# A short bias table, sums shared between two engines, first MLP products in the last attention pair, and identity products on TensorE

## The chip, the cores and the metric

The kernel runs on one core of a Trainium2 chip. The metric is the device time of one execution in microseconds (us), smaller is better. TensorE (PE in the rows) multiplies; PEld is its weight load. VectorE (DVE), ScalarE (ACT) and GpSimd (POOL) work element by element, SyncE (SP) issues transfers. Each has its own instruction stream, executed in order; they meet at semaphores.

## What is computed

A banded attention followed by two MLPs, all in float32. The reference, cut:

```python
# q, k, v: (2, 8, 768, 64); n_global 8, n_local 96
scores = scale * q @ k^T - slope[head] * dist       # dist: distance in the band, n_local for the global columns
scores = where(is_global | is_local, scores, -1e9)
x = softmax(scores) @ v                              # then (1536, 512)
h = x @ w_in                                         # w_in (512, 2048)
x = (h * tanh(softplus(h))) @ w_out                  # w_out (2048, 512)
for e in range(4):                                   # 4 experts, w1 (512, 1024), w2 (1024, 512)
    out += p[:, e:e+1] * (relu(x @ w1[e]) @ w2[e])
```

## The kernel before

**Attention** takes about the first sixth of the time. Its 16 heads form 8 pairs; a pair has 12 units, one for each of 6 blocks of 128 queries and each head, so there are 96 units, counted 0 to 95. Unit `u` goes through five steps:

1. scores: PE, `scores_of_two` (L535), for two units at once, three units ahead of the unit in hand. For the first block of queries a unit has 128 key columns, for the second 256, for the others 288.
2. bias, scale and running minimum: DVE, `biased` (L1074), two units ahead. It adds the table `dist_b` that `band_tables` (L1047) makes at the start: distance to the key plus a huge negative number where the key is masked.
3. exponential: ACT, `expo` (L824), two units ahead.
4. transpose: PE, `turn` (L566), then a high part by ACT (L858) and a low part by DVE (L1184).
5. product with the values: PE, `pv` (L585), two units behind.

After 6 units the outputs are divided by their sums and stored in `acc` (DVE, `output`, L1106 to L1114). While a pair runs, q and k of the next are transposed: PE, `fill` (L497), in four parts at units 0, 2, 4 and 6 of the pair, each copied out of one PSUM bank by ACT (`copy_out`, L814 and L817). The order is q tiles 0 to 3, q tiles 4 and 5, k tiles 0 to 3, k tiles 4 and 5. Before unit 0 the same is done for pair 0, and its scores wait for all four copies.

Beside this, in the same streams: DVE takes the largest absolute value of the values of each pair (`value_step`, L1155, units 0 to 6) and makes a scale from it (unit 7). ACT sums the absolute values of `w_in` in 8 pieces of 128x1024 at units 21 to 28, and of `w_out` at units 33 to 40 (`weights_sum`, L841). DVE makes scales of these (`matrix_scale`), and POOL splits both matrices into two float16 parts (L745 to L751).

**The first MLP** has 48 steps T (3 groups g of 512 tokens, 16 blocks of w_in columns). `first_product(T)` is 12 products of 128x512 (L635) in bank T % 4. Then ACT and DVE form the activation: ACT L939; DVE L1297, L1299, L1303 on the same T; ACT L953, L955 and DVE L1315, L1317 on T-1; POOL L790; ACT L947 and DVE L1309 on T-2. `second_product(T - 4)` is 12 products (L658). Before all this PE transposes the attention output: for g = 0 inside the last four pairs, for g = 1 and 2 in `turn_x` (L505, 16 transposes), at the steps that the table `TURN_AT` gives; ACT and DVE then take high and low parts (ACT L893, DVE `x_low`, L1169, 4 each). `second_product(0)` writes to the banks that `turn_x` used, so it waits until all of `x_low` is done. `first_product(0)` waits for the last `output` of attention. The experts follow.

The order in every stream is written out in the program; nothing is rearranged.

Of the kernel before, what the change touches and what calls it, by code (L numbers as in the profile page):

```python
# [13 lines left out]
P = 128  # L14
# [22 lines left out]
def program(nc, q, k, v, n_global, n_local, w_in, w_out, probs, w1, w2, out):  # L37
# [35 lines left out]
    with ExitStack() as ctx:  # L73
# [103 lines left out]
        dist_b, key_b, loc_b = (scratch(BAND_COLS) for _ in range(3))  # L177
# [5 lines left out]
        rel_b, glo_b = dist_b, tmp[:, 3 * BAND_COLS:4 * BAND_COLS]  # L183
# [56 lines left out]
        w_piece = sem("w_piece")  # L240
# [56 lines left out]
        TURN_AT = {0: 1, 2: 2}  # L297
# [39 lines left out]
        FILL = [(j, t) for j in range(2) for t in (range(HEAD), range(HEAD, QT))]  # L337
# [38 lines left out]
        def run_attention(eng, first, pair, rest):  # L376
# [18 lines left out]
            with eng.If(banded == 1):  # L395
                run(True)
                rest()
            with eng.Else():
                run(False)
                rest()  # L400
# [79 lines left out]
        def _(pe):  # L480
            def fill(i, slot, k, banded):
# [14 lines left out]
                for n, t in enumerate(tiles):  # L496
                    last = pe.transpose(psum(k if m_0 else 3, P, n * P), nat[slot][j][:, t * P:(t + 1) * P], ident[:])  # L497
# [10 lines left out]
            def score_parts(i, slot, u, banded):  # L508
# [3 lines left out]
                if u == 0:  # L512

                    pe.wait_ge(tr_out, FILLS * (2 * i + slot + 1))
# [73 lines left out]

            def pair(i, slot, banded):
                for u in range(UNITS):  # L590
# [34 lines left out]
            def rest():  # L625

                pe.wait_ge(o_ready, 2 * PAIRS + 2)

                def split_product(dst, lhs, rhs, chunks, fresh=None):

                    for c in range(chunks):
                        if fresh is not None:
                            fresh(c)
                        for n, (a, b) in enumerate(((0, 0), (0, 1), (1, 0))):
                            last = pe.matmul(dst, lhs(c, a), rhs(c, b), start=(c == 0 and n == 0),  # L635
                                             stop=(c == chunks - 1 and n == 2))
                    return last

                def first_product(T):

                    g, f = divmod(T, FT)
                    if T >= 4:
                        pe.wait_ge(b_ready, T - 3)
                    split_product(psum(T % 4), lambda c, s: w_in_s[:, s, c, f * P:(f + 1) * P],
                                  lambda c, s: xs(g, c, s), DC).then_inc(h_psum, 1)
# [51 lines left out]
                pe.wait_ge(x_ready, DC)  # L697
                pe.wait_ge(w_split, 1)
                for T in range(STEPS + LAG):
                    if T < STEPS:  # L700
# [3 lines left out]
                    if T in TURN_AT:  # L704
                        pe.wait_ge(x_ready, DC * TURN_AT[T])
# [13 lines left out]
            pe.wait_ge(ident_ready, 1)  # L719
            for k in range(FILLS):  # L720
# [85 lines left out]
        def _(act):  # L806
# [27 lines left out]
            def weights_sum(n, c):  # L834
# [3 lines left out]
                if n + c:  # L838
                    act.wait_ge(w_piece, PIECES * n + c)
                src = w_out_raw if n else stage  # L840
                act.activation(scaled[:], src[:, c * PIECE:(c + 1) * PIECE], ACT.Abs,  # L841
                               accum_out=wpieces[:, c:c + 1]).then_inc(w_piece, 1)
# [7 lines left out]
            def pair(i, slot, banded):  # L850
                for u in range(UNITS):
# [568 lines left out]
```

## Time and profile before

| what | us |
|---|---|
| median of 3 runs (lowest, highest) | 916.49 (912.8, 917.21) |
| the profiled execution, its own time | 915.88 |
| its span in the trace | 913.8 |
| attention, until the last product with the values | 153 |
| from there to `first_product(5)` | 24 |
| the rest, MLP and experts | 737 |

The trace was taken from one execution. In a row, a time in us comes first, then the duration, the engine, the line, the operation and the tiles; what stands in brackets is the idle time of the engine just before it and what ended that. The granted clock of PE (PEclk) is 1.00 at 2.4 GHz and 0.50 at 1.2 GHz. Float32 products are seen twice in the trace for each one in the program.

### The profile page before, as it was taken

The numbers are of one execution on the slowest core, as the hardware profiler recorded it, in microseconds if no ns is written. First come the engines' busy times: TensorE is split into PE (matmuls) and PEld (weight loads), VectorE is DVE, ScalarE is ACT, GpSimd is POOL, SyncE is SP. The second block draws the span as 40 slices with busy tenths as digits, with TensorE's granted clock in tenths as the row PEclk, the third lists the DMA queues.
The fourth block names the chain that finished last, engine by engine and source line by source line (L and its number), as shares of the span: only waits on it lengthen the run. The fifth ranks groups of instructions, "written<-read, shape, count | busy, mean of one in ns | idle before, by whom it ended". The sixth has DMA issues, their size and how long they took to land.

```text
span 913.8 us, 12568 instructions
## 1 busy us (share of the span) xinstructions
PE 873.1 (96%) x4884; PEld 441.3 (48%) x4884; DVE 506.8 (55%) x1016; ACT 315.7 (35%) x591; POOL 266.0 (29%) x218
## 2 busy tenths in 40 slices
PE   3878998999999999999999999999999999999998
PEld 3766786444444444444444444444444444444443
DVE  7855876999999999996642225322134322212121
ACT  3699885545454555454030111101020101101020
POOL 1266994122222232320009500059000193000000
PEclk8798999999999999999999999999999999999999
DMA  9762340000000000202000400000400000000001
GB/s 220 242 220 55 82 156 1 1 1 1 0 1 10 1 0 1 78 18 93 4 6 0 151 34 0 7 1 2 182 1 0 6 0 0 1 24 23 34 12 49
DMA packets 52005, 39.20 MB, mean 43 GB/s; under 512 B 40816, under 2 KB 41712, under 8 KB 51440
## 3 DMA queue, kind: packets, MB, share of 16 engines
q1 hardware_dynamic: 49888, 34.31, 12.5%
q10 hardware_dynamic: 2064, 4.19, 1.3%
q8 instruction: 31, 0.51, 0.3%
q14 instruction: 22, 0.18, 0.1%
HBM read 35.35 MB, written 3.15 MB: 42 GB/s over the span
## 4 chain that ended last, share of the span: by engine, by line
PE 69%; DVE 21%; ACT 7%; issue 2%; DMA 0%; POOL 0%; DVEq 0%; SPq 0%; ACTq 0%
PE bank L635 58%; PE bank L658 5%; DVE tmp L1299 4%; DVE tmp L1317 3%; PE bank L540 2%; DVE xT L1315 2%; DVE tmp L1297 2%; PE bank L566 2%; DVE tmp L1303 2%; ACT scaled L841 2%; PE bank L585 1%; DVE hid L1309 1%; ACT tmp L824 1%; ACT tmp L858 1%; ACT tmp L953 1%
## 5 line engine op out<-in xcount | busy, mean ns | idle before, releaser
L927 ACT ACTIVATE hid<-bank 128x512 f16<-128x512 f32 x96 | 57.3, 596 | 410.6 <-PE bank L635 410.6
L635 PE MATMUL bank<-xT,wA 128*128 128x512 f16 (+1 forms) x864 | 196.2, 381 | 1.1 <-DVE acc L1114 1.1
L1290 DVE SCALAR_TENSOR_TENSOR hid<-bank,hid 128x512 f16<-128x512 f32 x96 | 66.4, 692 | 172.3 <-ACT hid L927 172.3
L658 PE MATMUL bank<-hid,wB 128*128 128x512 f16 x576 | 132.2, 379 | 4.4 <-ACT acc L911 2.6
L635 PEld LDWEIGHTS bank<-xT,wA 128*128 128x128 f16 x864 | 84.8, 98 | 103.7 <-issue 2.2
L790 POOL TENSOR_TENSOR tmp<-tmp 128x512 f32<-128x512 f32 x48 | 70.1, 1460 | 198.2 <-DVE tmp L1317 198.2
L635 PE MATMUL bank<-wA,hid 128*128 128x512 f16 x576 | 125.3, 379 | 0.0
L635 PE MATMUL bank<-xT,wB 128*128 x576 | 125.3, 379 | 0.0
L635 PE MATMUL bank<-wB,hid 128*128 128x512 f16 x576 | 125.3, 379 | 0.0
L745 POOL TENSOR_SCALAR stage<-stage,sc 128x1024 f32<-128x1024 f32 x32 | 35.9, 1120 | 252.8 <-DVEq L1283 240.8
L1366 DVE SCALAR_TENSOR_TENSOR acc<-bank,pg,acc 128x512 f32<-128x512 f32 x36 | 27.0, 751 | 131.7 <-PE bank L635 131.7
L658 PEld LDWEIGHTS bank<-hid,wB 128*128 128x128 f16 x576 | 56.1, 98 | 73.0 <-DVE hid L1309 3.6
L635 PEld LDWEIGHTS bank<-wA,hid 128*128 128x128 f16 x576 | 56.4, 98 | 67.9
L635 PEld LDWEIGHTS bank<-xT,wB 128*128 128x128 f16 x576 | 56.4, 98 | 68.0
L635 PEld LDWEIGHTS bank<-wB,hid 128*128 128x128 f16 x576 | 56.4, 98 | 68.0
L947 ACT ACTIVATE hid<-tmp 128x512 f16<-128x512 f32 x48 | 30.2, 630 | 107.8 <-POOL tmp L790 106.0
L1184 DVE SCALAR_TENSOR_TENSOR tmp<-bank,tmp 128x384 f16<-128x384 f32 (+2 forms) x96 | 47.0, 490 | 30.5 <-ACT tmp L858 29.4
L635 PE MATMUL bank<-xT,hid 128*128 (+1 forms) x288 | 63.3, 379 | 0.0
L824 ACT ACTIVATE tmp<-tmp 128x288 f32<-128x288 f32 (+2 forms) x96 | 48.7, 507 | 20.3 <-DVE tmp L1074 18.8
L566 PE MATMUL bank<-ident,tmp 128*128 128x128 f32 x240 | 47.4, 299 | 6.0 <-DVE tmp L1184 3.3
L1299 DVE SCALAR_TENSOR_TENSOR tmp<-tmp 128x512 f32<-128x512 f32 x48 | 48.4, 1007 | 1.6
L540 PE MATMUL bank<-hid 64*128 64x256 f32 (+2 forms) x320 | 39.7, 360 | 9.1 <-DVE tmp L1074 8.2
(110 smaller groups left out, 930.6 us busy)
## 6 DMA issues: line engine op xcount, KB each, us to landing
stage<-in_moe_w SPq DMA_DIRECT2D x8, 2048.0 KB, 9.1
stage<-in_moe_w_in SPq DMA_DIRECT2D x1, 4096.0 KB, 14.2
wB<-in_moe_w_out ACTq DMA_DIRECT2D x1, 4096.0 KB, 15.9
hid<-in_q SPq DMA_DIRECT2D x16, 192.0 KB, 3.2
hid<-in_k SPq DMA_DIRECT2D x16, 192.0 KB, 3.4
xT<-in_v SPq DMA_DIRECT2D x8, 384.0 KB, 5.1
out_y<-acc SPq DMA_DIRECT2D x12, 256.0 KB, 2.0
rows<-max SPq DMA_DIRECT2D x4, 128.0 KB, 4.2
```

What stands on the lines that cost most here:

```text
L540: last = pe.matmul(*parts[a][n], start=True, stop=True)
L566: last = pe.transpose(dst[:, b * P:(b + 1) * P], src[:, b * P:(b + 1) * P], ident[:])
L635: last = pe.matmul(dst, lhs(c, a), rhs(c, b), start=(c == 0 and n == 0), stop=(c == chunks - 1 and n == 2))
L658: last = pe.matmul(psum(4 + d), w_out_s[:, a, f // 2, f % 2, d * P:(d + 1) * P], hv[:, T % RING, b, :], start=(f == 0 and n == 0), stop=(f ...
L745: pool.tensor_scalar(tmp, src, scale, 1.0, ALU.mult, ALU.mult).then_inc(w_part, 1)
L790: pool.tensor_tensor(g_t[T % 4], g_t[T % 4], r_t[T % 2], ALU.mult).then_inc(g_ready, 1)
L824: act.activation(t, t, ACT.Exp, bias=nmax[:, u:u + 1], scale=-1.0).then_inc(p_ready, 1)
L927: act.activation(hv[:, f, 0, :], psum(f % 4), ACT.Relu).then_inc(f_hi, 1)
L947: act.activation(hv[:, m % RING, 0, :], g_t[m % 4], ACT.Copy).then_inc(h_hi, 1)
L1184: dve.scalar_tensor_tensor(pt[:, 1], src, P_SCALE, pt[:, 0], ALU.mult, ALU.subtract).then_inc(pT_dve, 1)
L1290: dve.scalar_tensor_tensor(hv[:, f, 1, :], psum(f % 4), 0.0, hv[:, f, 0, :], ALU.max, ALU.subtract).then_inc(f_ready, 1)
L1299: dve.scalar_tensor_tensor(n, u, 2.0, u, ALU.add, ALU.mult).then_inc(n_ready, 1)
```

## The change

- **Short table.** `band_tables` loses its helper `distances`: one operation of 128x672 and three memsets of the score buffers now stand ahead of the wait for `bounds`, and four operations of 128x672 behind it where there were eight.
- **Start.** PE multiplies the identity 13 times (`keep_busy`) as soon as it exists. `FILL` now orders its parts q 0 to 3, k 0 to 3, q 4 and 5, k 4 and 5 (in every pair), and the scores of pair 0 wait only for the first two copies. `biased` of unit 2 is moved ahead of the value scale; `value_step(0)` ahead of the low part of the values.
- **Shared sums.** Of the 8 pieces of each weight matrix ACT keeps the even ones, DVE takes the odd ones (`weights_part`, one reduction of 128x1024). Of the 7 reductions of values DVE keeps four, and ACT takes those of pairs 3, 5 and 7 at units 2, 4 and 6.
- **First MLP products in the last pair.** At units 9, 10 and 11 of pair 7 PE does half of `first_product(0)`, its other half, and half of `first_product(1)`, 6 products each. The wait for the last `output` is moved from ahead of the MLP to ahead of `turn_x`. `TURN_AT` puts the transposes of g = 1 behind step 1 (was 0) and those of g = 2 behind step 3 (was 2).
- **Identity products.** In `scores_of_two` for units 6 to 46 PE multiplies the identity by itself three times, behind the waits of the scores and ahead of the scores, in the bank that the scores then overwrite: 21 places, 63 products.

```diff
-        dist_b, key_b, loc_b = (scratch(BAND_COLS) for _ in range(3))
+        dist_b, key_b = (scratch(BAND_COLS) for _ in range(2))
...
-        TURN_AT = {0: 1, 2: 2}
+        TURN_AT = {1: 1, 3: 2}
+        EARLY = [(0, (0, 1)), (0, (2, 3)), (1, (0, 1))]
...
+        V_SUMS = list(range(3, PAIRS, 2))
         W_SUMS = ({0: 21, 1: 33}, {0: UNITS})
+        BUSY = range(6, W_SUMS[0][1] + PIECES + 6)
...
-        FILL = [(j, t) for j in range(2) for t in (range(HEAD), range(HEAD, QT))]
+        FILL = [(j, t) for t in (range(HEAD), range(HEAD, QT)) for j in range(2)]
...
-                if u == 0:
-
+                if banded and before(i, slot) is None:
+                    if u in (0, 2 * HEAD):
+                        pe.wait_ge(tr_out, 2 if u == 0 else FILLS)
+                elif u == 0:
                     pe.wait_ge(tr_out, FILLS * (2 * i + slot + 1))
...
                 parts = [score_parts(i, slot, u + a, True) for a in range(2)]
+                if (2 * i + slot) * UNITS + u in BUSY:
+                    for _ in range(3):
+                        pe.matmul(psum(u % 3, P), ident[:], ident[:], start=True, stop=True)
...
+            def keep_busy(times):
+                for _ in range(times):
+                    pe.matmul(psum(3, P), ident[:], ident[:], start=True, stop=True)
...
                     scores_of_two(0, 0, 2)
+                    keep_busy(3)
...
+                        if not after(i, slot) and u >= UNITS - len(EARLY):
+                            n = u - (UNITS - len(EARLY))
+                            if n == 0:
+                                pe.wait_ge(x_ready, DC)
+                                pe.wait_ge(w_split, 1)
+                            first_product(*EARLY[n])
                         if behind:
                             pv(*behind, banded)
...
-                pe.wait_ge(o_ready, 2 * PAIRS + 2)
...
                 for T in range(STEPS + LAG):
-                    if T < STEPS:
+                    if banded and T < 2:
+                        if T:
+                            first_product(1, (2, 3))
+                    elif T < STEPS:
                         first_product(T)
                     else:
                         expert_first(0, 0, T - STEPS)
                     if T in TURN_AT:
+                        pe.wait_ge(o_ready, 2 * PAIRS + 2)
                         pe.wait_ge(x_ready, DC * TURN_AT[T])
...
             pe.wait_ge(ident_ready, 1)
+            keep_busy(13)
...
-                        if start <= at < start + PIECES:
+                        if at - start in range(0, PIECES, 2):
...
+                    if at + 1 in V_SUMS:
+                        values_sum(at + 1)
...
+            dve.wait_ge(iotas, 3)
+            dve.scalar_tensor_tensor(rel_b, rel_b, -1.0e9, rel_b, ALU.mult, ALU.max)
+            for s in s_b:
+                last = dve.memset(s[:, 2 * P + GLOBAL_COLS:3 * P], 0.0)
+            link(last)
...
-                distances(link, rel_b, key_b, loc_b, glo_b)
-                link(dve.tensor_scalar(loc_b, loc_b, -1.0, 1.0e9 * 2 ** H / SCALE, ALU.add, ALU.mult))
-                dve.scalar_tensor_tensor(dist_b, rel_b, -1.0 / SCALE, loc_b, ALU.mult, ALU.add).then_inc(band_ready, 1)
+                link(dve.tensor_scalar(key_b, key_b, bf[:, 0:1], -1.0e9 * 2 ** H / SCALE, ALU.is_ge, ALU.mult))
+                link(dve.scalar_tensor_tensor(key_b, rel_b, bf[:, 1:2], key_b, ALU.is_ge, ALU.mult))
+                link(dve.tensor_scalar(rel_b, rel_b, bf[:, 1:2], -1.0 / SCALE, ALU.min, ALU.mult))
+                dve.tensor_tensor(dist_b, rel_b, key_b, ALU.add).then_inc(band_ready, 1)
...
+                    if first is not None and at - first in range(1, PIECES, 2):
+                        weights_part(n, at - first)
```

On PE, the end of attention and the beginning of the MLP. `bank<-ident,tmp` is `turn`, the 128x65 products are `pv`, `bank<-xT,wA` is `first_product`, `bank<-ident,acc` is `turn_x`, `bank<-hid,wB` is `second_product`. Before:

```order
L566 MATMUL bank<-ident,tmp 128x128 x3
L585 MATMUL bank<-xT,tmp 128x65 x27
L635 MATMUL bank<-xT,wA 128x512 x12
L505 MATMUL bank<-ident,acc 128x128 x16
L635 MATMUL bank<-xT,wA 128x512 x24
L505 MATMUL bank<-ident,acc 128x128 x16
L635 MATMUL bank<-xT,wA 128x512 x24
L658 MATMUL bank<-hid,wB 128x512 x12
```

Now, from unit 9 of the last pair on:

```order
L581 MATMUL bank<-ident,tmp 128x128 x3
L610 MATMUL bank<-xT,wA 128x512 x6
L600 MATMUL bank<-xT,tmp 128x65 x9
L581 MATMUL bank<-ident,tmp 128x128 x3
L610 MATMUL bank<-xT,wA 128x512 x6
L600 MATMUL bank<-xT,tmp 128x65 x27
L610 MATMUL bank<-xT,wA 128x512 x6
L509 MATMUL bank<-ident,acc 128x128 x16
L610 MATMUL bank<-xT,wA 128x512 x24
L509 MATMUL bank<-ident,acc 128x128 x16
L610 MATMUL bank<-xT,wA 128x512 x12
L679 MATMUL bank<-hid,wB 128x512 x12
```

Three half products moved in among the last units, and of the products that stood behind the second `turn_x` only one is left behind it.

On ACT, from unit 20 to 24, where the pieces of `w_in` are summed. Before:

```order
L858 ACTIVATE tmp<-bank 128x384
L824 ACTIVATE tmp<-tmp 128x288
L841 ACTIVATE scaled,wpieces<-stage 128x1024
L858 ACTIVATE tmp<-bank 128x384
L824 ACTIVATE tmp<-tmp 128x128
L841 ACTIVATE scaled,wpieces<-stage 128x1024
L858 ACTIVATE tmp<-bank 128x384
L824 ACTIVATE tmp<-tmp 128x128
L841 ACTIVATE scaled,wpieces<-stage 128x1024
```

Now:

```order
L893 ACTIVATE tmp<-bank 128x384
L852 ACTIVATE tmp<-tmp 128x288
L868 ACTIVATE scaled,wpieces<-stage 128x1024
L893 ACTIVATE tmp<-bank 128x384
L852 ACTIVATE tmp<-tmp 128x128
L893 ACTIVATE tmp<-bank 128x384
L852 ACTIVATE tmp<-tmp 128x128
L868 ACTIVATE scaled,wpieces<-stage 128x1024
```

Every second piece left this stream; it stands in DVE's, behind the low part (L1237 now) of the same unit.

On PE, at unit 13, the scores of units 16 and 17 (`bank<-hid`). Before:

```order
L497 MATMUL bank<-ident,hid 128x128 x4
L566 MATMUL bank<-ident,tmp 128x128
L540 MATMUL bank<-hid 128x256 x2
L540 MATMUL bank<-hid 128x32 x2
L585 MATMUL bank<-xT,tmp 128x65 x9
```

Now:

```order
L501 MATMUL bank<-ident,hid 128x128 x4
L581 MATMUL bank<-ident,tmp 128x128
L546 MATMUL bank<-ident 128x128 x3
L549 MATMUL bank<-hid 128x256 x2
L549 MATMUL bank<-hid 128x32 x2
L600 MATMUL bank<-xT,tmp 128x65 x9
```

The three identity products stand between the transpose of the unit and the scores; everything behind them in the stream comes later by their length, if PE had no wait there.

## Rows read from the trace of the kernel before

**Rows 1.** The page, part 1: busy time, share of the span, instructions.

```profile
PE 873.1 (96%) x4884; PEld 441.3 (48%) x4884; DVE 506.8 (55%) x1016; ACT 315.7 (35%) x591; POOL 266.0 (29%) x218
```

**Rows 2.** Timeline, start of the program: start, duration, engine, line, operation, idle before.

```profile
3.03 0.28 DVE L1005 TENSOR_SCALAR ident<-tmp 128x128 f32<-128x128 f32 x1
...
6.61 0.51 DVE L1040 TENSOR_SCALAR tmp<-tmp 128x672 f32<-128x672 f32 x1 [1.04 <-issue]
7.15 0.92 DVE L1041 SCALAR_TENSOR_TENSOR tmp<-tmp,bf 128x672 f32<-128x672 f32 x1
...
7.63 2.79 PE L497 MATMUL bank<-ident,hid 128*128 128x128 f32 x12 [7.63 <-DMA hid<-in_k]
...
10.95 0.49 PE L540 MATMUL bank<-hid 64*128 64x128 f32 x4 [0.52 <-ACT hid L817]
...
12.34 0.86 DVE L1052 SCALAR_TENSOR_TENSOR tmp<-tmp 128x672 f32<-128x672 f32 x1
...
13.87 0.29 DVE L1074 CUSTOM_DVE_ANT_0 tmp<-bank,tmp 128x128 f32<-128x128 f32 x1 [0.23 <-DVE tmp L1384]
```

**Rows 3.** Groups of 0 to 154 us by form: count, busy us, mean ns, idle before.

```profile
L841 ACT ACTIVATE scaled<-stage 128x1024 f32<-128x1024 f32 x8 | 8.5, 1056 | 0.0
...
L1155 DVE TENSOR_REDUCE vpart<-xT 128x1 f32<-128x768 f32 x7 | 6.6, 943 | 0.0
```

**Rows 4.** Timeline, DVE, low part of units 12, 21, 29, 33 and 41.

```profile
40.43 0.29 DVE L1184 SCALAR_TENSOR_TENSOR tmp<-bank,tmp 128x128 f16<-128x128 f32 x1 [0.64 <-ACT tmp L858]
...
51.59 0.55 DVE L1184 SCALAR_TENSOR_TENSOR tmp<-bank,tmp 128x384 f16<-128x384 f32 x1
...
66.54 0.56 DVE L1184 SCALAR_TENSOR_TENSOR tmp<-bank,tmp 128x384 f16<-128x384 f32 x1 [0.91 <-ACT tmp L858]
...
71.22 0.55 DVE L1184 SCALAR_TENSOR_TENSOR tmp<-bank,tmp 128x384 f16<-128x384 f32 x1
...
87.06 0.56 DVE L1184 SCALAR_TENSOR_TENSOR tmp<-bank,tmp 128x384 f16<-128x384 f32 x1 [0.91 <-ACT tmp L858]
```

**Rows 5.** Timeline, PE: one float32 product, and the same scores two pairs apart.

```profile
69.86 0.47 PE L547 MATMUL bank<-ident,sc 128*128 128x128 f32 x2
70.16 0.49 PE L566 MATMUL bank<-ident,tmp 128*128 128x128 f32 x3
...
110.63 0.84 PE L540 MATMUL bank<-hid 64*128 64x256 f32 x8
...
139.37 0.84 PE L540 MATMUL bank<-hid 64*128 64x256 f32 x8
```

**Rows 6.** Stretches: from:to, length, PE busy (records), granted clock, DMA share, GB/s.

```profile
24.00:26.00 2.00, 2.00 (x21) 0.50 0.44 98
...
80.00:82.00 2.00, 2.00 (x8) 0.50 0.04 8
...
96.20:139.30 43.10, 40.65 (x525) 1.00 0.36 117
```

**Rows 7.** Timeline, PE and DVE, end of attention to step 5 of the MLP.

```profile
152.53 0.43 PE L585 MATMUL bank<-xT,tmp 128*128 128x65 f16 x9 [0.49 <-DVE tmp L1184]
...
154.04 4.43 PE L635 MATMUL bank<-xT,wA 128*128 128x512 f16 x12 [1.08 <-DVE acc L1114]
...
159.29 0.43 DVE L1297 TENSOR_SCALAR tmp<-tmp 128x512 f32<-128x512 f32 x1 [5.05 <-ACT tmp L939]
...
171.54 2.48 DVE L1169 TENSOR_TENSOR xT<-bank,xT 128x512 f16<-128x512 f32 x4
...
174.08 2.76 PE L658 MATMUL bank<-hid,wB 128*128 128x512 f16 x12 [1.75 <-DVE xT L1169]
...
176.68 2.75 PE L635 MATMUL bank<-xT,wA 128*128 128x512 f16 x12
...
177.65 0.42 DVE L1297 TENSOR_SCALAR tmp<-tmp 128x512 f32<-128x512 f32 x1
...
182.50 0.42 DVE L1297 TENSOR_SCALAR tmp<-tmp 128x512 f32<-128x512 f32 x1
```

More of the change, by code:

```diff
@@ L496, in fill @@
                 for n, t in enumerate(tiles):
-                    last = pe.transpose(psum(k if m_0 else 3, P, n * P), nat[slot][j][:, t * P:(t + 1) * P], ident[:])
+                    last = pe.transpose(psum(4 + k if m_0 else 3, P, n * P), nat[slot][j][:, t * P:(t + 1) * P], ident[:])
                 last.then_inc(tr_psum, 1)
@@ L587, in pv, with split_product, first_product @@
                 last.then_inc(pv_done, 1)
+            def split_product(dst, lhs, rhs, chunks, fresh=None, only=None):
+                for c in only or range(chunks):
+                    if fresh is not None:
+                        fresh(c)
+                    for n, (a, b) in enumerate(((0, 0), (0, 1), (1, 0))):
+                        last = pe.matmul(dst, lhs(c, a), rhs(c, b), start=(c == 0 and n == 0),
+                                         stop=(c == chunks - 1 and n == 2))
+                return last
+            def first_product(T, only=None):
+                g, f = divmod(T, FT)
+                if T >= 4:
+                    pe.wait_ge(b_ready, T - 3)
+                last = split_product(psum(T % 4), lambda c, s: w_in_s[:, s, c, f * P:(f + 1) * P],
+                                     lambda c, s: xs(g, c, s), DC, only=only)
+                if not only or DC - 1 in only:
+                    last.then_inc(h_psum, 1)
             def pair(i, slot, banded):
@@ L623, in pair, with rest @@
                     share_max(1)
-            def rest():
-                pe.wait_ge(o_ready, 2 * PAIRS + 2)
[L629 to L645, printed above, removed]
+            def rest(banded):
                 def second_product(T):
@@ L883, in pair @@
                     act.wait_ge(w_max, 1)
-                    for c in range(PIECES):
+                    for c in range(0, PIECES, 2):
                         weights_sum(1, c)
@@ L893, in x_high, with rest @@
                 act.activation(xs(g, c, 0), psum(x_bank(g, c)), ACT.Copy).then_inc(x_hi, 1)
-            def rest():
+            def rest(banded):
                 def x2_high(g, c):
@@ L1150, in value_step @@
             def value_step(u):
-                if u + 1 < PAIRS:
-                    n = u + 1
+                n = u + 1
+                if n < PAIRS and n not in V_SUMS:
                     dve.wait_ge(v_loaded[n], 16)
@@ L1178, in pair @@
                         biased(i, slot, u, banded)
-                    elif ahead:
+                    elif ahead and ahead != (0, 0, 2):
                         biased(*ahead, banded)
@@ L1208, in attention @@
                                   apply_absolute_value=True).then_inc(v_max, 1)
+                if is_banded:
+                    biased(0, 0, 2, is_banded)
                 dve.wait_ge(v_amax, 1)
@@ L1211, in attention @@
                 dve.sem_inc(v_scale, 1)
+                value_step(0)
                 values_low(0)
-                pair(0, 0, is_banded, value_step)
+                pair(0, 0, is_banded, lambda u: u and value_step(u))
                 pair(0, 1, is_banded, lambda u: matrix_step(1, u, is_banded))
@@ L1378, in _ @@
             with dve.If(banded == 1):
-                link = chain(table_step)
-                dve.wait_ge(iotas, 3)
-                band_tables(link)
+                band_tables(chain(table_step))
                 dve.wait_ge(band_ready, 1)
-                for s in s_b:
-                    last = dve.memset(s[:, 2 * P + GLOBAL_COLS:3 * P], 0.0)
-                link(last)
                 attention(True)
@@ L1392, in _ @@
                 dve.sem_inc(tables_free, 1)
+                for c in range(1, PIECES, 2):
+                    weights_part(1, c)
                 weights_max(1)
```

45 lines of the change are left out of this document (29 added, 16 removed).

## The prediction, made before the changed kernel ran

> **What bounds the kernel now.** I read the page's busy times first. TensorE is busy for 873 of 914 us [rows 1]; the change touches nothing behind step 5 of the MLP, at 177 us, and from there PE runs without a break. So the question is only how much earlier or later `first_product(5)`, now at 176.68 [rows 7], begins. I then read the timeline of the first 180 us and, beside it, the stretches with PE's granted clock. The reader is to see four different limits.
>
> In the start (0 to 14 us) DVE is the limit: PE could score at 10.95, DVE takes up the first scores at 13.87, when its table is done [rows 2]. In pair 0 DVE and a PE at 1.2 GHz share it: in 24 to 26 us PE is busy all the time at 0.50 [rows 6]. In the units in which weights are summed ACT is the limit: DVE waits 0.91 us for ACT's copy at units 29 and 41 [rows 4]. From pair 4 on PE is: two pairs take 28.74 us, 14.37 each or 2.40 for two units [rows 5], and PE is busy for 40.65 of 43.10 us [rows 6]. At the beginning of the MLP DVE is the limit: `second_product(0)` waits 1.75 us for `x_low` [rows 7].
>
> **Start and pair 0.** Removed behind the wait for the bounds: four of eight table operations. What is left is 0.51 + 0.92 + 0.51 + 0.86 = 2.80 us [rows 2], about 2.95 with gaps, instead of 7.26 (6.61 to 13.87). The operation put ahead costs 0.86, and the memsets are there too; half of it fits in DVE's wait for the bounds, the rest delays the flag by an estimated 0.3. DVE could take scores at 6.9 + 2.95 + 0.3 = 10.2. Now PE is late: 13 products seen twice are 26 records; the first 12 transposes took 2.79 us, 0.23 each [rows 2], so from 3.35 they last until 8.5 to 9.4, while k landed at 7.6. Eight transposes and two copies by ACT follow; scores at 10.2 to 11.3, DVE at 10.7 to 11.7. I take 10.9: -3.0 us.
>
> Then DVE loses three reductions, 3 x 0.94 = -2.8 [rows 3], which ACT gets, and PE gets five calls of the identity products. What one call costs: the one full float32 product of the trace holds PE for 0.30 us from its start to the next (69.86 to 70.16), of which some is the step over to it; as a stream two records of 128 columns should take 0.22, as transposes do. So 0.66 a call, 0.90 at most at full clock, about double at half clock, and nothing where PE waits anyway. Five calls: +3.3, partly under waits for DVE. If they keep the clock up they return more than that: PE is at 0.50 in much of pair 0 [rows 6]. The net from this to unit 14 I put at -2.0 (+1 to -4). Together **-5.0** (-2 to -7).
>
> Here the row and a rule meet. PE was busy for 2.00 of 2.00 us at a granted 0.50 in 24 to 26 us, with transposes among its records [rows 6]. The Trainium skill (TensorE: Matmul & The Clock Gate, Part 4: PE-mode transpose) says that a transpose does not count as busy for the clock as a plain product does. By that rule the identity products do what the transposes don't, the clock is up from an early call on, and the term would be the -7 of its lower end, the forecast 2 us lower.
>
> **Shared sums, units 21 to 28 and 33 to 40.** Now 66.54 - 51.59 = 14.95 and 87.06 - 71.22 = 15.84 us, 30.8 for 16 units, 3.85 for two [rows 4]. Of two pieces (1.06 us each [rows 3]) ACT loses one: 2.79 for two units, if only ACT counted. PE needs 2.40 [rows 5] + 0.66 = 3.06. DVE gets one reduction of 128x1024, 0.94 x 1024/768 = 1.25, on top of what it does for two units; it is the chain's other link and not far below 3. Three engines with about the same load never run at the bare sum: I take 3.25, so 8 x 3.25 = 26.0: **-4.8** (22.3 with hidden products, -8.5; nothing gained, 0). What stretched 80 to 82 us (clock 0.50 [rows 6]) is in the 15.84.
>
> **Identity products elsewhere.** Of 21 calls 5 are in pair 0 and 8 in the units just counted. The other 8 (issued in units 13 to 19, 29, 31, 41 and 43) come where PE has no wait to hide them: 51.59 - 40.43 = 11.16 us for units 12 to 20 is 2.48 for two units, PE's own pace [rows 4, 5]. 8 x 0.66 = **+5.3** (0 to 7.2). Queued behind them on PE: scores, `pv` and the next `turn`; DVE and ACT wait for these.
>
> **First products in the last pair.** PE gets 18 products of 0.217 us (174.08 to 176.68 for 12 [rows 7]), 3.9 us, at units 9 to 11. I estimate its idle time there at 1.4 us, from pauses like the 0.49 before the last `pv` [rows 7], so the last `pv` ends 2.5 us later. Behind it the stream is shorter: `first_product(0)` at 154.04 took 4.43 us, at full clock it is 2.75 [rows 7]. But PE does not set the end of this stretch, DVE does. DVE began step 0 at 159.29, which is 6.3 us after the last `pv` (152.96). Now steps 0 and 1 are ready by then, and DVE begins 2.1 us after it (the last `output`, two scale operations, ACT's exponential): 152.96 + 2.5 + 2.1 = 157.6, 1.7 earlier. From there to the end of `x_low` for g = 2 DVE was busy nearly without a gap, 159.29 to 174.02, 14.7 us [rows 7]. `TURN_AT` moves those transposes from step 2 to step 3, so one more step of DVE's work stands ahead of them: in 14.7 us less two `x_low` of 2.48 stand two and a half steps, 3.9 each; later steps follow each other in 4.85 (177.65 to 182.50), waits included. I take 3.9. Then 157.6 + 14.7 + 3.9 = 176.2 instead of 174.02, +2.2. PE, which now ends `first_product(4)` some 7 us before, waits all that time instead of 1.75, and after such a pause restarts at 1.2 GHz, as it did at 154.04 after 1.08: 4.43 - 2.75 = +1.7. Together **+4.0** (if the last pair hides everything and the extra step costs half, -2; if the restart costs double, +5.7). Nothing later gives it back, since PE runs without a pause from `second_product(0)` on.
>
> POOL's splits come earlier with the units and are not waited for. The new `FILL` order moves two transposes from unit 4 to unit 2 of a pair: 0.
>
> **Sum.** -5.0 - 4.8 + 5.3 + 4.0 = -0.5: 915.88 becomes 915.4. The median lay 0.6 above the profiled execution, so 916.0.
>
> **Rivals.**
> 1. *The products hide* (faster). The scores are issued three units ahead, so a delay of 0.66 need not reach anyone; the sums then go at 2.8 to 3.0 for two units, pair 0 at full clock. -7 - 7.5 + 2 + 4 = -8.5: 908. For it: in the summing units PE waits. Against it: in pairs 4 to 6 PE has only 2.45 of 43.10 us free [rows 6].
> 2. *PE becomes the bound of pairs 0 to 3* (slower). A call costs 0.90 and every one of the 21 is paid; the sums gain only 2. Pair 0 -2, sums -2, elsewhere +7.2, MLP +5.5: +8.7, 925. It decides once a call is over 0.8 us and two units with sums over 3.6.
> 3. *The identity products do not raise the clock* (the change does not do what it says). Pair 0 and the region of 80 us stay at 0.50, where a call costs 1.3. Pair 0 -2, sums -2.5, elsewhere +5.3, MLP +4: +4.8, 921.
> 4. *The long wait ahead of `second_product(0)` does not come*, since ACT and DVE overlap the extra step: MLP -1 instead of +4, the rest as forecast: 911.
>
> **How the numbers follow.** Forecast 916 (912 to 920): 0.47. Rival 1, 908: 0.17. Rival 4, 911: 0.11. Rival 3, 921: 0.10. Rival 2, 925: 0.15. The range 908 to 923 leaves out half of rival 1 and most of rival 2. A measurement can tell about 0.5%, 4.6 us, from no change: below 911.9 lie rivals 1 and 4, faster 0.28; same 0.47; above 921.1 rival 2 and most of rival 3, slower 0.25.
>
> **What would show it.** The first `biased` at 10.7 to 11.7 us. Unit 12's low part at about 35.5 (40.43 now). Units 21 to 28 in 13 us, units 12 to 20 in about 14. No 0.50 in the stretches between 30 and 150 us. A call of six records lasting 0.6 to 0.7 us. The wait of `second_product(0)` for `x_low` grown to about 7 us with the clock at 0.50 behind it, and `first_product(5)` at 176. I am wrong if the scores come no later for the calls, if the extra step of DVE is hidden, or if the clock falls in spite of them.

## The result, and the profile after

| | before | after |
|---|---|---|
| median, us (lowest, highest) | 915.96 (912.8, 917.21), 7 runs | 921.77 (921.2, 923.99), 7 runs |
| profiled execution, its own time | 915.88 | 922.25 |
| its span | 913.8 | 920.4 |

The changed kernel takes 1.0076 times as long, with a 95% interval of 1.0060 to 1.0091: slower by 7 us. The forecast was 916.0, no change. The time lies above the 912 to 920 that stood beside the forecast and inside the wider range of 908 to 923; the slowdown itself was missed.

In the profile after, lines 1237, 1123, 852, 893 and 868 are what 1184, 1074, 824, 858 and 841 were before. New are L1074 (a piece of a weight matrix, reduced by DVE) and L546 (the identity products). Part 1 of the page answers [rows 1]:

```profile
PE 885.5 (96%) x5042; PEld 456.4 (50%) x5042; DVE 504.7 (55%) x1018; ACT 312.7 (34%) x581; POOL 265.3 (29%) x218
```

PE has 158 records more, 126 of them the identity products ahead of the scores and 32 those at the start, and is busy for 12 us more. DVE and ACT have less to do than before, so no busy time says where the 7 us went. The timeline of the start answers [rows 2] (start, duration, engine, line, operation, idle before):

```profile
3.37 5.00 PE L562 MATMUL bank<-ident 128*128 128x128 f32 x26 [3.37 <-DVE ident L1042]
...
10.73 0.29 DVE L1123 CUSTOM_DVE_ANT_0 tmp<-bank,tmp 128x128 f32<-128x128 f32 x1 [0.85 <-PE bank L549]
```

The first scores are taken up at 10.73 instead of 13.87. The low parts of units 12, 21, 29, 33 and 41 answer [rows 4]:

```profile
36.51 0.29 DVE L1237 SCALAR_TENSOR_TENSOR tmp<-bank,tmp 128x128 f16<-128x128 f32 x1 [0.26 <-ACT tmp L893]
...
49.27 0.56 DVE L1237 SCALAR_TENSOR_TENSOR tmp<-bank,tmp 128x384 f16<-128x384 f32 x1
...
66.08 0.55 DVE L1237 SCALAR_TENSOR_TENSOR tmp<-bank,tmp 128x384 f16<-128x384 f32 x1
...
71.58 0.55 DVE L1237 SCALAR_TENSOR_TENSOR tmp<-bank,tmp 128x384 f16<-128x384 f32 x1
...
89.59 0.55 DVE L1237 SCALAR_TENSOR_TENSOR tmp<-bank,tmp 128x384 f16<-128x384 f32 x1
```

Differences of such rows (DVE's low part of the first and the last unit named) give the table that every experiment below is read with. In us:

```
units            before   after   difference
0 to 14           23.93   23.93    0.00   (unit 0 itself: 19.55, now 15.62)
14 to 21           8.11    9.72   +1.61
21 to 29 (sums)   14.95   16.81   +1.86
29 to 33           4.68    5.50   +0.82
33 to 41 (sums)   15.84   18.01   +2.17
41 to 48           8.98   10.14   +1.16
48 to 95          55.80   57.36   +1.56   (early products in the last pair)
```

So of the 3.93 us won at unit 0 and still there at unit 14, 0.46 are left at unit 29, and unit 48 comes at 99.73 instead of 96.04. The units in which DVE and ACT now share the sums should have become 4.8 us shorter and became 4.0 us longer. The end of attention and the MLP's first steps on PE answer [rows 7]:

```profile
157.66 0.99 PE L600 MATMUL bank<-xT,tmp 128*128 128x65 f16 x27
158.49 1.46 PE L610 MATMUL bank<-xT,wA 128*128 128x512 f16 x6
...
179.14 5.30 PE L679 MATMUL bank<-hid,wB 128*128 128x512 f16 x12 [6.34 <-DVE xT L1222]
184.23 3.00 PE L610 MATMUL bank<-xT,wA 128*128 128x512 f16 x12
```

`second_product(0)` waits 6.34 us for `x_low`, where it waited 1.75, and its 12 products take 5.30 us, where 2.76 is full clock. The stretches from 176 us on (from:to, length, PE busy with its records, granted clock, DMA share, GB/s) show the clock at its lower level, 1.2 GHz, behind that pause:

```profile
176.00:178.00 2.00, 0.00 (x0) 0.97 0.00 0
178.00:180.00 2.00, 0.86 (x3) 0.50 0.00 0
180.00:182.00 2.00, 2.00 (x6) 0.50 0.01 4
```

`first_product(5)` begins at 184.23 instead of 176.68: 7.55 us late, of which 3.69 stem from before unit 48 and 3.86 from here.

**The ring.** Why did less work for ACT make the sum units longer? The chain of waits of both kernels tells it. Before, from 53.66 us on (start, us, what):

```profile
53.66 0.29 ACT tmp L824
53.95 1.04 ACT scaled L841 x2
54.99 0.37 ACT tmp L858
55.36 0.29 ACT tmp L824
55.65 1.04 ACT scaled L841 x2
```

The chain never leaves ACT: exponential, a piece (1.04), copy, 1.7 us a unit. After, the same stretch:

```profile
55.60 1.21 DVE wpieces L1074
56.81 0.26 issue
57.19 0.51 ACT tmp L852
57.70 0.57 ACT hid L842
58.27 1.04 ACT scaled L868 x2
59.31 0.28 ACT tmp L893
59.65 0.30 issue
59.96 1.21 DVE wpieces L1074
```

The chain now goes round between the two engines, and it holds DVE's piece and ACT's piece, one behind the other: 4.36 us for two units (55.60 to 59.96), 1.21 + 1.04 of it the two reductions. The timeline shows the two waits that close the ring:

```profile
57.19 0.51 ACT L852 ACTIVATE tmp<-tmp 128x256 f32<-128x256 f32 x1 [1.26 <-DVE tmp L1123]
...
58.17 1.05 ACT L868 ACTIVATE scaled<-stage 128x1024 f32<-128x1024 f32 x1
...
59.62 0.42 DVE L1237 SCALAR_TENSOR_TENSOR tmp<-bank,tmp 128x256 f16<-128x256 f32 x1 [1.81 <-ACT tmp L893]
...
59.96 1.21 DVE L1074 TENSOR_REDUCE wpieces<-stage 128x1 f32<-128x1024 f32 x1
```

In units 22, 24 and so on, those of the odd pieces, DVE's reduction stands ahead of `biased` for a unit ahead, and ACT idles for 1.26 us. In the unit between, ACT's piece stands ahead of its copy, and DVE idles for 1.81 us. Each engine does its piece while the other waits for it. Below this is called theory R (the ring). Its rival is theory P, that PE with its identity products is the bound.

### The profile page after: what moved, and what is told of

It is laid out like the page before. It is cut to its first block, busy times and chain, and to the rows that moved or that the text cites. A ratio compares the mean times of both kernels' runs of the same rounds, so it can differ in the third digit from the quotient of the medians.

```text
span 920.4 us, 12884 instructions
## 1 busy us (share of the span) xinstructions
PE 885.5 (96%) x5042; PEld 456.4 (50%) x5042; DVE 504.7 (55%) x1018; ACT 312.7 (34%) x581; POOL 265.3 (29%) x218
## 3 DMA queue, kind: packets, MB, share of 16 engines
HBM read 35.35 MB, written 3.15 MB: 42 GB/s over the span
## 4 chain that ended last, share of the span: by engine, by line
PE 84%; DVE 9%; ACT 4%; issue 2%; SPq 1%; DMA 0%; POOL 0%; DVEq 0%; ACTq 0%
PE bank L610 65%; PE bank L679 12%; PE bank L549 2%; PE bank L581 2%; PE bank L600 2%; DVE tmp L1353 1%; DVE tmp L1355 1%; ACT scaled L868 1%; ACT tmp L852 1%; PE bank L501 1%; ACT tmp L893 1%; DVE xT L1222 1%; SPq L418 1%; DVE tmp L1373 1%; DVE tmp L1359 1%
## 5 line engine op out<-in xcount | busy, mean ns | idle before, releaser
L679 PE MATMUL bank<-hid,wB 128*128 128x512 f16 x576 | 134.7, 384 | 7.8 <-DVE xT L1222 6.3
L773 POOL TENSOR_SCALAR stage<-stage,sc 128x1024 f32<-128x1024 f32 x32 | 35.9, 1123 | 253.3 <-DVEq L1339 241.0
L1237 DVE SCALAR_TENSOR_TENSOR tmp<-bank,tmp 128x384 f16<-128x384 f32 (+2 forms) x96 | 47.0, 490 | 28.5 <-ACT tmp L893 27.4
L976 ACT ACTIVATE tmp<-bank,sc 128x512 f32<-128x512 f32 x48 | 32.8, 685 | 56.4 <-PE bank L610 53.3
L581 PE MATMUL bank<-ident,tmp 128*128 128x128 f32 x240 | 44.6, 285 | 7.3 <-DVE tmp L1237 4.9
L1353 DVE TENSOR_SCALAR tmp<-tmp 128x512 f32<-128x512 f32 x48 | 39.5, 823 | 13.3 <-ACT tmp L976 13.2
## 6 DMA issues: line engine op xcount, KB each, us to landing
stage<-in_moe_w_in SPq DMA_DIRECT2D x1, 4096.0 KB, 14.7
```

The costliest lines, as they stand in the source:

```text
L581: last = pe.transpose(dst[:, b * P:(b + 1) * P], src[:, b * P:(b + 1) * P], ident[:])
L679: last = pe.matmul(psum(4 + d), w_out_s[:, a, f // 2, f % 2, d * P:(d + 1) * P], hv[:, T % RING, b, :], start=(f == 0 and n == 0), stop=(f ...
L773: pool.tensor_scalar(tmp, src, scale, 1.0, ALU.mult, ALU.mult).then_inc(w_part, 1)
L976: act.activation(u_t[T % 2], psum(T % 4), ACT.Exp, scale=inv_h).then_inc(u_ready, 1)
L1237: dve.scalar_tensor_tensor(pt[:, 1], src, P_SCALE, pt[:, 0], ALU.mult, ALU.subtract).then_inc(pT_dve, 1)
L1353: dve.tensor_scalar(u, u, U_MAX, None, ALU.min).then_inc(n_step, 1)
```

## The experiments

Kernels that were measured together share one set of runs of the kernel before. The ratio to that set is given with each, and kernels of different sets are compared by their ratios. The kernels whose names begin with a_ are the changed kernel with one part edited. The places of units are read from one trace of each kernel.

### Without the identity products ahead of scores (a_noident)

```diff
-        BUSY = range(6, W_SUMS[0][1] + PIECES + 6)
+        BUSY = range(0)
```

> The changed kernel without the 21 calls of three identity products ahead of scores; the 13 and the 3 of the start stay. Theory R (ring): in units 21 to 28 and 33 to 40 ACT's piece and DVE's reduction stand in units that follow each other and lie one behind the other in one ring of waits, so both are paid in full; the identity products are hidden there. Then these 16 units stay at 34.8 us, only the other stretches lose about 3.6, and the time is about 918. Theory P (PE): the identity products make PE the bound there too; the 16 units fall to 28 us or less and the time to 909 to 911.

Measured: 918.29 us, 1.0049 of before (1.0026 to 1.0072), span 915.1. The sum units took 16.79 and 17.99 us, as with the products (16.81, 18.01). Units 14 to 21, 29 to 33 and 41 to 48 took 8.03, 4.83 and 9.48, together 3.02 less. So the products are hidden where the ring turns and are paid in the other units behind unit 14; PE is not what made the sum units long, as theory R has it. Units 0 to 14 took 21.17 instead of 23.93; more on that under d_pair0.

### The same products alone, on the kernel before (b_ident)

```diff
                 parts = [score_parts(i, slot, u + a, True) for a in range(2)]
+                if (2 * i + slot) * UNITS + u in range(6, 47):
+                    for _ in range(3):
+                        pe.matmul(psum(u % 3, P), ident[:], ident[:], start=True, stop=True)
```

> The kernel before with nothing but the 21 calls of three identity products. Theory R: hidden in the 16 units, where ACT alone sums (30.8 us stay, less 1 or 2 if the clock stays up at 80 us); paid elsewhere, some 3.6 us in units 12 to 47 and 1 to 3 in pair 0 where PE runs at half clock; time about 920. Theory P: 16 units at 34 us or more, time 924 or above.

Measured: 918.42 us, 1.0046 (1.0026 to 1.0065), span 915.4. Sum units 14.96 and 15.85, unchanged. Units 0 to 14 +0.52, 14 to 21 +1.84, 29 to 33 +0.66, 41 to 48 +0.65: unit 48 at 99.72, 3.68 later. The edit costs the kernel before about as much up to unit 48 as the whole change does. Of those 3.7 us about 2 did not reach the end of the span (+1.6): `first_product(0)` ran at the upper clock there, 2.76 us for its 12 products where [rows 7] have 4.43. That need not come from the products. Behind the same wait of 1.07 or 1.08 us these 12 products took 4.43 to 4.45 us in three traces (before, a_noearly, d_start) and 2.76 or 2.77 in two (b_ident, d_noearly), and a_noearly has the identity products too.

### All pieces of the weights on ACT again (a_actsums)

```diff
-                        if at - start in range(0, PIECES, 2):
+                        if at - start in range(PIECES):
...
-                    if first is not None and at - first in range(1, PIECES, 2):
-                        weights_part(n, at - first)
```

> The changed kernel with all 16 pieces of the weight sums on ACT, as in the kernel before, and none on DVE; values stay shared, identity products stay. Theory R: the 16 units go back to the 30.8 us of before, time about 918. Theory P: with PE as the bound it makes no difference or is worse (ACT has more to do), 34.8 us or more, time 921 or above.

Measured: 917.39 us, 1.0036 (1.0025 to 1.0047), span 916.1. Sum units 15.07 and 15.97, within 0.13 of what they were before, with the identity products still there. Undoing the sharing alone gives back 3.7 us (1.0076 less 1.0036): the sharing is what costs, not what stands around it.

### DVE's piece in the same unit as ACT's (a_sameunit)

```diff
-                    if first is not None and at - first in range(1, PIECES, 2):
-                        weights_part(n, at - first)
+                    if first is not None and at - first in range(0, PIECES, 2):
+                        weights_part(n, at - first + 1)
```

> The changed kernel with DVE's reduction moved from the unit behind ACT's piece into the same unit, so that the two lie side by side. Theory R: the ring pays one of the two instead of both, 1.0 to 1.2 us less for two units; the 16 units take 26 to 28 us instead of 34.8, time about 914. Theory P: no change, 921.

Measured: 913.16 us, 1.0000 (0.9984 to 1.0016), span 911.2. Sum units 12.50 and 13.70: 26.2 us where the changed kernel has 34.8 and the kernel before 30.8. No operation was added or taken away; four pieces of each matrix moved by one unit. The timeline of this kernel shows the pieces side by side:

```profile
53.03 1.04 ACT L868 ACTIVATE scaled<-stage 128x1024 f32<-128x1024 f32 x1
53.07 1.21 DVE L1074 TENSOR_REDUCE wpieces<-stage 128x1 f32<-128x1024 f32 x1
...
55.56 1.21 DVE L1074 TENSOR_REDUCE wpieces<-stage 128x1 f32<-128x1024 f32 x1
...
56.19 1.05 ACT L868 ACTIVATE scaled<-stage 128x1024 f32<-128x1024 f32 x1
```

With the pieces side by side two units take 26.2 / 8 = 3.27 us. That is close to the 3.25 of the forecast, but not for the forecast's reason, which was the load of PE with its identity products. Up to unit 29 the chain of waits goes on between ACT and DVE, with one piece for two units instead of two, and enters PE only at 60.95 us, 0.9 us before the low part of unit 29. An estimate from the rows fits: the ring took 16.81 / 4 = 4.20 us for two units up to there, less ACT's piece of 1.05 that is 3.15; measured are 12.50 / 4 = 3.12. And c_three below, which has no identity products here, takes the same 12.50.

Of these 8.6 us, 7.6 arrive at unit 48 (92.09 for 99.73), since units 29 to 33 and 41 to 48 took 0.9 more. The ratio fell from 1.0076 to 1.0000, 7.0 us. The fall of the clock at 80 us is gone too: 1.00 from 74 to 90 us, where the changed kernel has

```profile
74.00:78.00 4.00, 2.20 (x30) 1.00 0.00 0
78.00:82.00 4.00, 3.95 (x30) 0.61 0.02 4
82.00:86.00 4.00, 4.00 (x23) 0.53 0.00 0
```

There PE was busy for 2.20 of 4.00 us, then the clock fell, in spite of the identity products among its records.

### The end of attention and the MLP as before (a_noearly)

```diff
-        TURN_AT = {1: 1, 3: 2}
+        TURN_AT = {0: 1, 2: 2}
-        EARLY = [(0, (0, 1)), (0, (2, 3)), (1, (0, 1))]
+        EARLY = []
...
+                pe.wait_ge(o_ready, 2 * PAIRS + 2)
...
-                    if banded and T < 2:
-                        if T:
-                            first_product(1, (2, 3))
-                    elif T < STEPS:
+                    if T < STEPS:
```

> The changed kernel with the end of attention and the start of the MLP as in the kernel before: no first products in the last pair, transposes behind steps 0 and 2. If the prediction's term for this part holds (+4.0 by its working), the wait for x_low is 1.75 us again, the clock stays up behind it, and the time is 3 to 4 us below the changed kernel, 918. Rival: the early products were worth something after all and the loss is only in attention: 921 to 923.

Measured: 919.45 us, 1.0044 (1.0031 to 1.0057), span 917.9. `first_product(5)` begins at 180.73, 3.5 us before that of the changed kernel:

```profile
158.08 4.45 PE L610 MATMUL bank<-xT,wA 128*128 128x512 f16 x12 [1.07 <-DVE acc L1160]
...
178.13 2.76 PE L679 MATMUL bank<-hid,wB 128*128 128x512 f16 x12 [1.74 <-DVE xT L1219]
180.73 2.75 PE L610 MATMUL bank<-xT,wA 128*128 128x512 f16 x12
```

The old order has its own fall of the clock (4.45 us for 12 products) and still gets there first. The wait is the 1.7 expected; the time lies between the 918 expected and the 921 of the rival.

### The second transposes behind step 2 (a_turn12)

```diff
-        TURN_AT = {1: 1, 3: 2}
+        TURN_AT = {1: 1, 2: 2}
```

> The changed kernel with the second group of transposes behind step 2 instead of step 3, early products kept. If the extra step of DVE ahead of x_low is what makes the long wait, the wait of 6.3 us ahead of second_product(0) is gone; instead PE waits some 4 us ahead of the second transposes (for the first x_low). first_product(5) comes 4.5 to 6.5 us earlier than at 184.2, time 915.5 to 917.5. Rival: the wait only moves ahead of the transposes in full and the clock falls there: 920 to 922.

Measured: 917.82 us, 1.0026 (1.0015 to 1.0037), span 916.1.

```profile
168.78 3.41 PE L509 MATMUL bank<-ident,acc 128*128 128x128 f32 x16 [3.98 <-DVE xT L1222]
171.99 5.58 PE L610 MATMUL bank<-xT,wA 128*128 128x512 f16 x24
177.41 2.75 PE L679 MATMUL bank<-hid,wB 128*128 128x512 f16 x12
180.00 2.75 PE L610 MATMUL bank<-xT,wA 128*128 128x512 f16 x12
```

The pause has moved ahead of the transposes and is 3.98 instead of 6.34 us. The slow clock behind it costs 1.5 us on the transposes (3.41 against 1.91), and `second_product(0)` waits for nothing. `first_product(5)` comes 4.2 us earlier, where 4.5 was the least expected, and the time is 0.3 above the range expected. The step that the change had put ahead of `x_low` is what the wait ahead of `second_product(0)` was made of; about 4 us of waiting for DVE are left, ahead of the transposes.

### PE kept at work through the wait (a_fillwait)

22 identity products into a free bank, in the pause ahead of `second_product(0)`:

```diff
                     if T == 0:
+                        pe.wait_ge(b_ready, 2)
+                        for _ in range(22):
+                            pe.matmul(psum(1, P), ident[:], ident[:], start=True, stop=True)
                         pe.wait_ge(x_ready, XN)
```

> The changed kernel with 22 identity products in the pause ahead of second_product(0). They take 22 x 0.28 = 6.1 us, what the pause lasts. If the fall of the clock in the pause costs what 5.30 instead of 2.75 us for its 12 products say, second_product(0) starts where it did (179.1) and first_product(5) 2.5 to 2.9 us earlier, time 919. Rival: identity products don't hold the clock in a pause, or the loss comes back later: 921 to 922.

Measured: 919.47 us, 1.0051 (1.0032 to 1.0070), span 917.9.

In this kernel L674 is the filler and L682 `second_product`. Its timeline:

```profile
172.75 5.07 PE L674 MATMUL bank<-ident 128*128 128x128 f32 x44
179.25 2.76 PE L682 MATMUL bank<-hid,wB 128*128 128x512 f16 x12 [1.43 <-DVE xT L1225]
181.85 2.75 PE L610 MATMUL bank<-xT,wA 128*128 128x512 f16 x12
```

The product starts no earlier (179.25, 179.14 in the changed kernel) but runs at the upper clock: the next begins 2.4 us earlier. So of the 3.86 us of this part about 2.4 are the clock behind the pause. The rest, about 1.4, is that `second_product(0)` itself begins later. The price of the clock is not a constant: behind the same wait of 6.33 us the 12 products took 5.30 us in a_noident, 4.93 in a_actsums and 4.33 in a_sameunit.

### Three edits together (c_three)

The edits of a_sameunit, a_noident and a_turn12 in one kernel.

> Three edits of the changed kernel together: reduction in the same unit as ACT's piece, no identity products ahead of scores, second transposes behind step 2. If the three are independent: 913.2 for the first, 4 to 5 less for the second, 4 to 6 less for the third, 903 to 905, below both kernels. Rival: without identity products ACT and DVE are the bound in the 16 units, or the clock falls in attention, and it is 907 to 910.

Measured: 904.83 us (903.92 to 907.0), 0.9892 of before (0.9862 to 0.9921), span 903.8. Sum units 12.50 and 14.25, unit 48 at 87.78 (96.04 before), unit 95 at 145.12 (151.84). It is 10 us faster than the kernel before and 17 us faster than the changed one, inside the 903 to 905 expected.

### The start part alone (d_start)

The changed kernel with the edits of a_noident, a_actsums and a_noearly: what is left of the change is the short table, the start, and the reductions of values that ACT takes from DVE.

> The changed kernel with three of its parts undone: no identity products ahead of scores, all weight pieces on ACT, the end of attention and the beginning of the MLP as before. What is left is the start part alone: the short table, the 13 and 3 identity products at the start, the new FILL order and the reductions of values shared between DVE and ACT. Theory (the start part is a plain gain, and the units behind it do not take it back): unit 14 at 37.7 to 38.9 us (before 43.48), sum units 15.0 and 15.9 as before, unit 48 at 90.3 to 91.5 (before 96.04), second_product(0) waits 1.7 us for x_low as before; median 5 us under the kernel before, ratio 0.994 to 0.995. Rival (DVE or ACT is only late elsewhere, since work stood in the shadow of the slow start): the gain at unit 14 is halved by unit 48; ratio 0.997 to 0.999.

Measured: 911.54 us, 0.9957 (0.9944 to 0.9970), span 910.0. Unit 0 at 15.91 (19.55), unit 14 at 39.71 (43.48), unit 48 at 92.20 (96.04), unit 95 at 148.18 (151.84). The 3.8 us of the start arrive whole at the end of the span. The ratio is a little above the 0.994 to 0.995 expected, and the rival is out. At unit 14 it is 0.8 later than I expected; the clock fell in pair 0 (0.50 from 34 to 38 us), which is a likely cause and was not tried alone.

### Identity products in pair 0 alone (d_pair0)

c_three with the products put back in units 6 to 13, four calls:

```diff
-        BUSY = range(0)
+        BUSY = range(6, 14)
```

> c_three with the identity products put back in pair 0 alone (units 6 to 13, four calls of three products). Theory (they cost PE time where PE is the limit and do not hold the clock there): units 0 to 14 take 24 to 25 us instead of 23.5, and the clock shows 0.50 between 17 and 38 us in some stretches; median 0.5 to 2 us above c_three, ratio 0.990 to 0.991. Rival (they hold the clock in pair 0, as meant): units 0 to 14 in 21 to 22 us with a clock of 1.00 after 20 us; 1.5 to 2.5 us below c_three, ratio 0.987.

Measured: 905.37 us, 0.9893 (0.9872 to 0.9914), no difference from c_three. The clock from 30 to 38 us, in one stretch, d_pair0 first and c_three behind it:

```profile
30.00:38.00 8.00, 6.25 (x84) 1.00 1.00 389
```

```profile
30.00:38.00 8.00, 7.28 (x69) 0.57 1.00 393
```

The same holds from 26 to 42 us in all kernels with this start. In the seven that have the products there (after, a_sameunit, a_actsums, a_noearly, a_turn12, a_fillwait, d_pair0) the mean granted clock is 1.00, and their products of 64x256 take 0.84 us for eight. In the four without (a_noident, c_three, d_start, d_noearly) it is 0.79 to 0.89. So here the products do hold the clock, and the prediction quoted a rule for that: the Trainium skill (TensorE: Matmul & The Clock Gate, Part 4: PE-mode transpose) says that a transpose does not count as busy as a plain product does. These records agree with it, but do not show it by themselves, since the products were added to the transposes and fill pauses too.

The time does not follow the clock. Units 0 to 14 take 23.73 to 23.93 us in the first six and 22.36 in d_pair0 (which has one call fewer by then), against 21.17, 21.87, 23.50 and 23.80 in those without. These four have one and the same program up to unit 20, and still differ by 2.6 us, so one trace of each can't say what the products cost here; it shows that they gain nothing. My expectation failed on the clock and was too high for the time; the rival was right on the clock and wrong on what it is worth.

### The old order of the MLP in the best kernel (d_noearly)

c_three with the end of attention and the MLP as in a_noearly.

> c_three with the end of attention and the beginning of the MLP as in the kernel before (no first products in the last pair, transposes of the turned x behind steps 0 and 2). Theory: the early first products together with transposes behind steps 1 and 2 are worth about 1.6 us against the old order, as the difference between a_noearly and a_turn12 was; so the median is 1 to 2 us above c_three, ratio to before 0.990 to 0.992, unit 95 at 143.6, second_product(0) waits 1.7 us. Rival (c_three's gain is in the sum units and the start alone, and the early products are worth nothing or cost): equal to c_three or below, ratio 0.989 or less.

Measured: 906.31 us, 0.9912 (0.9882 to 0.9942), span 902.8. By the ratios it is 1.8 us slower than c_three, with intervals that overlap, by the spans 1.0 faster. In its trace `second_product(0)` begins at 162.93 instead of 164.92, of which 1.18 is already there at unit 48.

The other 0.8 is the clock at `first_product(0)`, which stayed up here (144.57 to 147.34, 2.77 us) and fell in the three other traces of the old order named under b_ident. From unit 48 to the end of the span d_noearly takes 816.2 us and b_ident 815.7; those three take 817.8 each; a_turn12 and c_three, with early products and the second transposes behind step 2, take 815.8 and 816.0, and d_pair0, with that order too, 817.1. So the early products are worth 0.7 to 2.0 us where the clock falls at `first_product(0)` without them, and nothing where it stays up. What decides between the two is open.

## Why the prediction was wrong

**The step that failed** is the term "Shared sums": -4.8 expected, +4.0 measured (34.82 us for 30.79), 8.8 us off and more than the whole error. Its sentence "I take 3.25" added up each engine's load for two units (ACT 2.79, PE 3.06, DVE not far below 3) and took the largest with a margin. That is right for engines that run beside each other. It did not ask in what order the two pieces come on the chain exponential, copy, low part, `biased`. By the chain of waits they came in series, and two units took 4.35 us. a_sameunit shows that the order was the cause: with the pieces side by side it is 3.27. That this is so near 3.25 is in part luck, since the forecast had PE's 3.06 as the largest load, and the first eight sum units take 12.50 us with the identity products (a_sameunit) and without them (c_three). a_actsums shows that nothing else was in it. The order of `weights_part` and `biased` on DVE could have been read from the changed kernel before it ran. Rival 2 had the right sign for the whole, but not for this term, where it too had a gain of 2, and the wrong engine: it made PE the bound, and a_noident shows PE's products hidden in just these units.

**A call of six records.** Forecast 0.66 us, 0.90 at most. Measured from the start of a call to the start of the scores behind it, 0.77 (59.03 to 59.80), and 1.42 at the lower clock:

```profile
18.72 1.49 PE L546 MATMUL bank<-ident 128*128 128x128 f32 x6
20.14 1.19 PE L549 MATMUL bank<-hid 64*128 64x256 f32 x8
```

**Identity products elsewhere.** +5.3 forecast, +3.6 measured in the whole change, and 3.0 of it vanish in a_noident. Each call was dearer than thought, but of the eight calls' 6.2 us (8 x 0.77) only about half arrived.

**Start and pair 0.** First `biased` at 10.73 for 10.9: right, -3.1. Unit 14 -3.9 for -5.0, unit 12 at 36.51 for 35.5. The rest of the way to unit 14 gained 0.8 instead of 2, all of it ahead of unit 0. The clock came up in pair 0 as the rule quoted in the prediction has it, but the -7 that the prediction worked out for that case did not come. How much of the miss is the calls stays open: with them units 0 to 14 took 22.36 to 23.93 us, without them 21.17 to 23.80.

**First products in the last pair.** +4.0 forecast, +3.86 measured, and right in its parts. The last `pv` came 2.0 us later than the shift of unit 48 explains (2.5 forecast). DVE began step 0 at 160.75, 2.1 us behind its end at 158.65 (2.1 forecast). From there to the end of `x_low` it took 18.3 us, 160.75 to 179.08 (14.7 + 3.9 = 18.6 forecast). The restart cost 2.5 us, 5.09 for 2.60 (1.7 forecast, with double as its bound). Rival 4 is out.

**The clock.** "No 0.50 between 30 and 150 us" failed: it fell at 78 to 86 us. Products or pauses alone do not decide it. With the products and without the ring (a_actsums, a_sameunit) it is 1.00 in every stretch from 42 to 96 us. With the products and the ring it fell behind 78 us, without the products and with the ring (a_noident) at 54 to 62 and 74 to 86 us. With neither it fell too: at 78 us in the kernel before, by 74 us in c_three, d_start, d_pair0 and d_noearly. In c_three (from:to, length, PE busy with its records, granted clock, DMA share, GB/s):

```profile
70.00:74.00 4.00, 3.15 (x26) 0.64 0.02 4
```

Rival 3 is half right: the products hold the clock in pair 0, and at 80 us only where the ring's pauses are gone.

**The sum.** -3.9 + 3.6 + 4.0 + 3.9 = +7.6 at `first_product(5)`. "Nothing later gives it back" was off by 1.0: the span grew by 6.6. The waits of PE (us in total, times, longest) show `second_product` waiting later for `acc`, twice and 2.6 us before, once and 1.5 us after. First before, then after:

```profile
PE bank L658 <- ACT acc L911: 2.6, 2, 2.2
```

```profile
PE bank L679 <- ACT acc L948: 1.5, 1, 1.5
```

That accounts for the size. It goes with the early products and the new `TURN_AT`: in a_noearly, which differs from the changed kernel in these alone, the wait is back, 2.8 us in two times. In all five traces of the old order it is 2.6 to 2.9 us in two times, in the eight of the new ones 1.4 to 1.8 in one.

## What to carry to other kernels

When side work is shared between two engines that hand tiles to each other in a chain, give both their piece in the same step: in alternate steps each does its piece while the other waits, and the chain holds both. The load of an engine per step is a lower bound only; read from the order of instructions what stands ahead of the operation that the other engine waits for. Filler products on PE are free only in steps where another engine holds the chain, so count the slack step by step, and where PE pauses, try to shorten the pause (a_turn12, 1.0026) and not only to fill it (a_fillwait, 1.0051).

## What the runs showed of the hardware

- Moving four reductions of 1.21 us per matrix by one unit, with no other change, made the 16 sum units 8.6 us shorter (34.8 to 26.2) and brought unit 48 7.6 us forward.
- 22 float32 products of 128x128, 44 records, kept PE at a granted 1.00 through a pause of 6.3 us, for 5.07 us of PE time; without them the next 12 products took 5.30 us instead of 2.76 (4.33 to 5.30 in four kernels with the same pause).
- The identity products between the scores kept the clock at 1.00 in pair 0. At 80 us they did so in the two kernels without the ring and not in the changed kernel, where PE was busy for 2.20 of 4.00 us.
- Behind a wait of 1.07 or 1.08 us the same 12 products took 4.43 to 4.45 us in three traces and 2.76 or 2.77 in two.
- The record of the granted clock can be missing: in b_ident it says 1.00 for 18 to 26 us, while eight products of 64x256, 0.84 us at the upper clock, took 1.49; the kernel before has the same 1.49 at 19.78 us, with 0.50 on record there. Durations of the same form are the safer reading:

```profile
19.77 1.49 PE L543 MATMUL bank<-hid 64*128 64x256 f32 x8 [2.85 <-DVE tmp L1077]
...
28.04 0.84 PE L543 MATMUL bank<-hid 64*128 64x256 f32 x8
```

- A reduction of 128x1024 by DVE took 1.21 us, ACT's pass with an accumulator over the same tile 1.05; the estimate of 1.25 from the 128x768 row was good.
